# A linear-attention layer and two MLPs on one core: VectorE turns k as well as r and w

## The chip, the core and the metric

The kernel runs on one core of a Trainium2 chip. The core has TensorE (matrix products), VectorE, ScalarE and GpSimd (elementwise work), SyncE (here it only issues transfers), and 16 DMA engines that carry them. The engines run independently and wait for each other by semaphores; within an engine everything happens in the order written. The metric is the time of one execution in microseconds (us), less is better; the median of several runs counts.

## The reference

Three parts follow each other. The first is a recurrence over 768 steps for 4 batches of 8 heads of size 48, the second a dense MLP on 3072 tokens of 384 values, the third a mixture of 8 experts of which every token uses one.

```python
state = np.zeros((B, H, D, D))
for t in range(S):
    kt, vt, rt, wt = (k[:, :, t], v[:, :, t], r[:, :, t], w[:, :, t])
    cur = np.einsum('bhd,bhe->bhde', u[None] * kt, vt)
    y[:, :, t] = np.einsum('bhd,bhde->bhe', rt, state + cur)
    state = wt[:, :, :, None] * state + np.einsum('bhd,bhe->bhde', kt, vt)
# y as x, (tokens, 384)
h = x @ w_in                      # 384 -> 2048
x2 = np.maximum(0.01 * h, h) @ w_out
# experts: xn, en are x2 and expert_emb, normalized
logits = xn @ en.T / tau          # the router: 8 logits per token
expert_idx = np.argmax(logits, axis=1)
# out = softmax weight * relu(x2 @ w1[e]) @ w2[e], e = expert_idx
```

## The kernel before

**The attention.** The recurrence is worked off in 24 chunks of 128 steps (six for each batch, all heads together), numbered m = 0 to 23 in the code; this text counts the first to the 24th. For a chunk r, k and w are loaded with time along the partitions and must be turned, so that head values lie along the partitions and time along the columns. From the turned w VectorE makes running products (`decay_to`: `Fi`) and suffix products (`decay_from`: `Xi`) by scans; `decay_rk` multiplies the turned r and k by them into `Rh` and `Kt`. TensorE multiplies `Kt` by `Rh` (`scores`), VectorE masks the result (`mask`), and TensorE sums it with v and with the carried state (`sums`). GpSimd multiplies r, k and u for the diagonal (`products(m)` in its block), VectorE sums these into `bonus`, and ScalarE writes the diagonal (`diagonal`, eight operations on `As`).

**Who turns.** TensorE turns a chunk of 128 x 512 by four products with the identity into a PSUM bank. VectorE's `transpose` turns only blocks of 32 x 32 in place, so for it the blocks must be placed by the load: `load_blocks` does that with 16 small transfers. From the sixth chunk on w goes that way, from the tenth (`R_BLOCKED` = 9) r does too, half of its transfers issued by ScalarE's queue. k is turned by TensorE in all chunks (`turn_rk`), right behind a feature product.

**The MLP.** Tokens go in eight groups of three chunks (384 tokens). A group has 16 slots, f = 0 to 15. In slot n TensorE runs `feature(n)` (nine products of 384 columns, L1085) and `out_part(n - 2)` (nine, L1106). Between them ScalarE copies the feature out (`feature_copy`: `gw`), VectorE applies the leak (`leak`), ScalarE rounds it (`feature_hi`: `gh`) and VectorE takes the rest (`feature_lo(n - 1)`: `gl`), which stands first in VectorE's slot n. In ScalarE's slot n `feature_hi(n - 1)` stands first, then `feature_copy(n)`, then `diagonal`.

**How the two are mixed.** The three chunks of the next group are worked off inside the slots of the current one, by a table written by hand. `SLOTS` gives for the first, second and third chunk the slots of w's turn, of r and k's turn, of the scores and of the sums: (-2, -1, 1, 3), (3, 4, 6, 8) and (8, 9, 11, 13); negative slots are those at the end of the group before. VectorE's `decay_rk` comes in the slot after the turn, 0, 5 and 10, right behind `gl`. `BLOCK_SLOTS` gives VectorE's turn of w, `decay_to` and `decay_from`. The 24 router products of a group (`products(first, G, ...)`, L1809: each multiplies 384 values by an expert's vector and sums them) stand at the end of VectorE's slots. Their number per slot comes from a rule: none in slots 3, 4, 9 and 14, three in slots without attention work just before, else two, and the rest in slot 15; that gives 2, 0, 0, 2, 3, 2, 2, 0, 2, 3, 2, 3, 0 for slots 2 to 14 and 3 for slot 15.

**SyncE.** It issues nearly all transfers, in the order of the slots: the block loads of w (`next_w`, 16 transfers), r (`next_r`, eight), the plain r and k (`next_load`), v, and at a group's end the copies that fill the holes between heads of 48 in rows of 64 (`fill`). The chunk's plain k has three buffers, `m % NSLOT`.

## Time and profile before

| | us |
|---|---|
| median of 3 runs | 825.2 |
| lowest and highest | 823.98, 826.25 |
| the profiled execution | 825.9 |
| its span | 824.1 |
| TensorE busy | 807.5 |
| VectorE busy | 566.3 |
| ScalarE busy | 439.0 |
| GpSimd busy | 203.9 |

The times of single instructions come from the profiled execution; its span is what the trace covers. The attention lies in the first 475 us, almost all of it inside the MLP's slots, the experts follow from about 543 us on. A busy TensorE is not one at its peak, since matmuls overlap; what counts is the distance of their starts. The granted TensorE clock is full all along. In a timeline row stand start, duration, engine, line, operation, the tiles written and read, shapes and count; in brackets the engine's idle time before it and what ended it.

### The profile page before, as it was taken

To read this page: it belongs to the slowest core of one execution; us is meant where nothing else is said; L and a number is where in the kernel's file an instruction comes from. 1 tells how busy PE (TensorE), PEld (TensorE's weight loads), DVE (VectorE), ACT (ScalarE), POOL (GpSimd) and SP (SyncE) were. 2 spreads that over 40 slices of the span, in tenths; PEclk is the share of its full clock that TensorE was granted. 3 is DMA by queue.
4 is the path that set the end of the run, shared out by engine and by line. 5 is a ranking of instruction groups with operands and counts; after the bars stand their busy time and mean duration, and the time that the engine had idled before them with its cause. 6 is when DMAs were issued, how large, how long until landed. Compare 5 with 4: busy or idle time off the path is not lost. (4 is left out here: it accounts for less than half of the span.)

```text
span 824.1 us, 18207 instructions
## 1 busy us (share of the span) xinstructions
PE 807.5 (98%) x5573; PEld 757.5 (92%) x5573; DVE 566.3 (69%) x1330; ACT 439.0 (53%) x924; POOL 203.9 (25%) x288
## 2 busy tenths in 40 slices
PE   6999999999999999999999999999999999999996
PEld 6899999999999999999999999999989888998886
DVE  6879787789889878979979855735541512455463
ACT  6676564464375375465465444663643533565473
POOL 5611111112003002103112002303542422434423
PEclk9999999999999999999999999999999999999999
DMA  9975431347344243243330012215432414386291
GB/s 205 207 155 132 75 76 27 58 87 92 64 75 55 45 88 49 44 91 51 50 72 14 1 41 87 100 39 183 147 98 78 155 48 124 103 287 205 85 309 56
DMA packets 199866, 81.51 MB, mean 99 GB/s; under 512 B 170046, under 2 KB 187813, under 8 KB 199650
## 3 DMA queue, kind: packets, MB, share of 16 engines
q1 hardware_dynamic: 173682, 66.79, 34.1%
q0 software_dynamic: 4544, 10.85, 4.1%
q10 hardware_dynamic: 21552, 2.81, 2.5%
q8 instruction: 42, 0.69, 0.4%
q14 instruction: 46, 0.38, 0.2%
HBM read 115.85 MB, written 11.63 MB: 155 GB/s over the span
## 5 line engine op out<-in xcount | busy, mean ns | idle before, releaser
L1085 PE MATMUL bank<-xhl,WRh 128*128 128x384 f32 x768 | 219.1, 339 | 0.4 <-issue 0.2
L1085 PEld LDWEIGHTS bank<-xhl,WRh 128*128 128x128 f32 x768 | 141.3, 188 | 1.1 <-issue 1.1
L1106 PE MATMUL bank<-WRh,gh 128*128 128x384 f32 x384 | 135.8, 354 | 0.0
L1085 PE MATMUL bank<-xhl,WRl 128*128 128x384 f32 x384 | 130.0, 339 | 0.0
L1106 PE MATMUL bank<-WRh,gl 128*128 128x384 f32 x384 | 129.8, 338 | 0.0
L1106 PE MATMUL bank<-WRl,gh 128*128 128x384 f32 x384 | 129.7, 338 | 0.0
L1466 ACT CAST gh<-gw 128x384 fp32r<-128x384 f32 x128 | 65.4, 511 | 105.6 <-DVE gw L1789 87.4
L1460 ACT COPY gw<-bank 128x384 f32<-128x384 f32 x128 | 61.5, 480 | 107.3 <-PE bank L1085 106.8
L1796 DVE TENSOR_TENSOR gl<-gw,gh 128x384 fp32r<-128x384 f32 x128 | 71.7, 560 | 58.7 <-ACT gh L1466 52.8
L1964 DVE TENSOR_TENSOR hl<-bank,hh 128x512 fp32r<-128x512 f32 x56 | 36.1, 686 | 84.3 <-ACT hh L1501 83.9
L1789 DVE SCALAR_TENSOR_TENSOR gw<-gw 128x384 f32<-128x384 f32 x128 | 73.3, 572 | 18.7 <-ACT gw L1460 18.7
L795 POOL TENSOR_TENSOR St<-Sx,FL 128x256 f32<-128x256 f32 x20 | 12.3, 615 | 280.3 <-DVE Sx L1770 218.2
L1809 DVE CUSTOM_DVE_ANT_0 junk<-x2s,embb 128x384 bf16<-128x384 f32 x144 | 74.4, 558 | 0.0
L1106 PEld LDWEIGHTS bank<-WRh,gh 128*128 128x128 f32 x384 | 72.2, 188 | 2.3 <-issue 0.7
L1942 DVE TENSOR_TENSOR WRl<-stage,WRh 128x1536 fp32r<-128x1536 f32 x36 | 62.0, 1755 | 16.1 <-ACT WRh L1474 15.2
L1106 PEld LDWEIGHTS bank<-WRl,gh 128*128 128x128 f32 x384 | 72.3, 188 | 0.0
L1085 PEld LDWEIGHTS bank<-xhl,WRl 128*128 128x128 f32 x384 | 72.2, 188 | 0.0
L1106 PEld LDWEIGHTS bank<-WRh,gl 128*128 128x128 f32 x384 | 72.1, 188 | 0.0
L1194 PE MATMUL bank<-WRh,hh 128*128 128x384 f32 x184 | 63.9, 347 | 1.3 <-DVEq L1953 1.3
L1509 ACT ACTIVATE os<-bank,gcol 128x384 f32<-128x384 f32 x28 | 16.3, 583 | 87.4 <-PE bank L1194 80.9
L1194 PE MATMUL bank<-WRl,hh 128*128 128x384 f32 x184 | 62.0, 337 | 0.0
L1194 PE MATMUL bank<-WRh,hl 128*128 128x384 f32 x184 | 61.9, 336 | 0.0
(202 smaller groups left out, 1633.8 us busy)
## 6 DMA issues: line engine op xcount, KB each, us to landing
stage<-in_moe_w_dram SPq DMA_DIRECT2D x96, 768.0 KB
Kn<-in_k_dram SPq DMA_DIRECT2D x24, 192.0 KB, 3.4
Vn<-in_v_dram SPq DMA_DIRECT2D x24, 192.0 KB
x_moe<-x2s SPq DMA_DIRECT2D x24, 192.0 KB, 3.8
Rn<-in_r_dram SPq DMA_DIRECT2D x21, 192.0 KB, 2.7
wraw<-in_moe_w_out_dram SPq DMA_DIRECT2D x4, 768.0 KB, 7.6
eraw<-in_moe_w_dram SPq DMA_DIRECT2D x4, 768.0 KB, 9.0
Wn<-in_w_dram SPq DMA_DIRECT2D x152, 16.0 KB
```

Of the source, the lines that this page charges most:

```text
L795: pool.tensor_tensor(St[:], Sx[:], FL[:, m % GT, :].unsqueeze(2).to_broadcast([P, HP, HEAD_PAD]), ALU.mult).then_inc(s_st, 1)
L1085: mm = pe.matmul(bank[F_BANK[n % 2]][:, 0:GN], win(t_)[:, f // 4, k_, cols], xhl[G % 2][:, a, k_, :], start=(k_ == 0 and n_ == 0), stop=(k ...
L1106: mm = pe.matmul(bank[O_BANK[i]][:, 0:DM], a[:, z, cols], wout(t_)[:, f, :], start=(f == 0 and n_ == 0), stop=(f == FT - 1 and n_ == 2))
L1194: mm = pe.matmul(bank[R_BANK[s_]][:, 0:DM], h_[:, f, :], w_[:, f, :], start=(f == 0 and n_ == 0), stop=(f == FT2 - 1 and n_ == 2))
L1460: act.copy(gw[:, n % 2, :], bank[F_BANK[n % 2]][:, 0:GN]).then_inc(s_g0, 1)
L1466: act.copy(gh[:, n % GS, :], gw[:, n % 2, :]).then_inc(s_ghi, 1)
L1509: act.activation(os[:, s_, :], bank[R_BANK[s_]][:, 0:DM], ACT.Copy, scale=gcol[:, s_, :]).then_inc(s_o2e, 1)
L1789: dve.scalar_tensor_tensor(gw[:, z, :], gw[:, z, :], 0.01, gw[:, z, :], ALU.mult, ALU.max).then_inc(s_g1, 1)
L1796: dve.tensor_tensor(gl[:, n % GS, :], gw[:, n % 2, :], gh[:, n % GS, :].bitcast(F32), ALU.subtract).then_inc(s_glo, 1)
L1809: dve.tensor_tensor_reduce(junk[:, m % 2, :], x2s[:, i, :], embb[:, e, :], 1.0, 0.0, ALU.mult, ALU.add, logits[:, GT * G + i, e:e + 1]).th ...
L1942: dve.tensor_tensor(sel(w1l, w2l), src, sel(w1h, w2h).bitcast(F32), ALU.subtract).then_inc(s_elo, 1)
L1964: dve.tensor_tensor(lo, bank[H_BANK[a]][:], hi.bitcast(F32), ALU.subtract).then_inc(s_hlo, 1)
```

## The change

From the thirteenth chunk on (`K_BLOCKED` = 12) TensorE no longer turns k. VectorE's `decay_rk` turns it by `turn_k` behind r. Its blocks come in two steps: in slots 18 to 33 of the whole run (groups two and three), 32 transfers copy k's second half, two batches, from DRAM to DRAM into `k_packed`; then each chunk's blocks are loaded by four transfers (`next_kb`) into the second and third of k's buffers, which GpSimd clears once. The plain k, still needed by GpSimd's product, from then on has only the first buffer and is loaded by `next_k` when the product before is done. VectorE's turn of w for the second chunk of a group moves from slot 0 to slot -1, and ScalarE's check of w's range with it. The router products get a table of their own, `SHARE`. The last two apply to earlier chunks as well.

```diff
+    k_packed = nc.dram_tensor("k_packed", [B * NCH // 2, 4, HP * 4, 32, 32], F32, kind="Internal").ap()
...
+        K_BLOCKED = B * NCH // 2
+        def k_slot(m):
+            return m % NSLOT if m < K_BLOCKED else 0
+        def k_blocks(m):
+            return 1 + m % 2
...
-        BLOCK_SLOTS = ((-5, -3, -2), (0, 2, 4), (6, 8, 9))
+        BLOCK_SLOTS = ((-5, -3, -2), (-1, 2, 4), (6, 8, 9))
+        SHARE = {2: 1, 3: 0, 4: 0, 5: 1, 6: 5, 7: 3, 8: 2, 9: 0, 10: 1, 11: 5, 12: 3, 13: 3, 14: 0}
...
                 load_one(sp, m, 1)
+                if m < K_BLOCKED:
+                    load_one(sp, m, 2)
+            def next_k(m):
+                sp.wait_ge(s_rk, m)
+                if m == K_BLOCKED:
+                    sp.wait_ge(s_kT, m - 2)
                 load_one(sp, m, 2)
+            def pack_k(h, a):
+                o, top = divmod(32 * a, HEAD_PAD)
+                n_ = min(32, D - top)
+                for b in range(B // 2):
+                    sp.dma_start(k_packed[b * NCH:(b + 1) * NCH, a, 4 * h:4 * h + 4, :, 0:n_].rearrange("c b j i -> (b j) c i"),
+                                 k[B // 2 + b, 2 * h + o, :, top:top + n_].rearrange("(c t) i -> t c i", t=P)
+                                 ).then_inc(s_packed, 16)
+            def next_kb(m):
+                sp.wait_ge(s_packed, 16 * 4 * HP * (B // 2))
...
+                for a in range(4):
+                    n_ = min(32, D - 32 * a % HEAD_PAD)
+                    to = Kn[32 * a:32 * a + 32, k_blocks(m)].rearrange("p h d -> p (h d)").rearrange("p (x i) -> p x i", i=32)
+                    sp.dma_start(to[:, :, 0:n_], k_packed[m - K_BLOCKED, a, :, :, 0:n_].rearrange("x j i -> j x i")
+                                 ).then_inc(s_kblk[m % 2], 16)
...
+                for m in at(turn_w_at, n):
+                    if K_BLOCKED <= m + 1 < NC:
+                        next_k(m + 1)
+                if FT + 2 <= n < FT + 2 + 4 * HP:
+                    pack_k(*divmod(n - FT - 2, 4))
...
                         for m in at(turn_at, n):
-                            turn_rk(m)
+                            if m < K_BLOCKED:
+                                turn_rk(m)
...
+            def turn_k(m):
+                dve.wait_ge(s_kblk[m % 2], 16 * 4 * ((m - K_BLOCKED) // 2 + 1))
+                dve.wait_ge(s_mk, m)
+                dve.transpose(bank[k_bank(m)][:], Kn[:, k_blocks(m)].rearrange("p h d -> p (h d)")).then_inc(s_kT, 1)
...
                 if m >= R_BLOCKED:
                     turn_r(m)
+                if m >= K_BLOCKED:
+                    turn_k(m)
...
-                        light = not any(at(t_, n - 1) for t_ in (turn_at, score_at, sum_at))
-                        some = 0 if f in (4, 9, 14) or (f == 3 and G > 1) else 3 if light and f != 8 else 2
+                        some = SHARE.get(f, 0)
```

TensorE's order behind the feature product of slot 15, at the turn of the 22nd chunk's k, before:

```order
L1085 MATMUL bank<-xhl,WRl 128x384
L1085 MATMUL bank<-xhl,WRh 128x384
L972 MATMUL bank<-ident,Kn 128x128 x4
L1106 MATMUL bank<-WRh,gh 128x384
L1106 MATMUL bank<-WRl,gh 128x384
```

and now (`feature` is L1146 there, `out_part` L1167):

```order
L1146 MATMUL bank<-xhl,WRl 128x384
L1146 MATMUL bank<-xhl,WRh 128x384
L1167 MATMUL bank<-WRh,gh 128x384
L1167 MATMUL bank<-WRl,gh 128x384
L1167 MATMUL bank<-WRh,gl 128x384
```

The four products with the identity are gone; nothing takes their place.

VectorE's order from the last `gl` of a group on, at the 19th chunk, before:

```order
L1796 TENSOR_TENSOR gl<-gw,gh 128x384
L1685 STREAM_TRANSPOSE bank<-Rn 128x512
L1736 TENSOR_TENSOR Rh<-bank,Fi 128x512
L1742 TENSOR_TENSOR Kt<-bank,Xi 128x512
L1789 SCALAR_TENSOR_TENSOR gw<-gw 128x384
L1679 STREAM_TRANSPOSE Wn<-Wn 128x512
```

and now, from the `gl` one slot earlier (`gl` is L1866, `leak` L1859, w's turn L1741, the turns of r and k L1747 and L1754):

```order
L1866 TENSOR_TENSOR gl<-gw,gh 128x384
L1859 SCALAR_TENSOR_TENSOR gw<-gw 128x384
L1741 STREAM_TRANSPOSE Wn<-Wn 128x512
L1866 TENSOR_TENSOR gl<-gw,gh 128x384
L1747 STREAM_TRANSPOSE bank<-Rn 128x512
L1754 STREAM_TRANSPOSE bank<-Kn 128x512
L1806 TENSOR_TENSOR Rh<-bank,Fi 128x512
L1812 TENSOR_TENSOR Kt<-bank,Xi 128x512
```

k's turn stands between r's and `Rh`; w's turn for the next chunk has moved ahead of `gl`, where three router products stood before.

VectorE's order in slot 6, between the 20th and the 21st chunk, from the `leak` to the next `gl`, before:

```order
L1789 SCALAR_TENSOR_TENSOR gw<-gw 128x384
L1679 STREAM_TRANSPOSE Wn<-Wn 128x512
L1809 ISA junk,logits<-x2s,embb 128x384
L1809 ISA logits 128x1
L1809 ISA junk,logits<-x2s,embb 128x384
L1809 ISA logits 128x1
L1809 ISA junk,logits<-x2s,embb 128x384
L1809 ISA logits 128x1
L1796 TENSOR_TENSOR gl<-gw,gh 128x384
```

and now, without the `leak` (the router products are L1879, each with a row that reads its sum):

```order
L1741 STREAM_TRANSPOSE Wn<-Wn 128x512
L1879 ISA junk,logits<-x2s,embb 128x384
L1879 ISA logits 128x1
L1879 ISA junk,logits<-x2s,embb 128x384
L1879 ISA logits 128x1
L1879 ISA junk,logits<-x2s,embb 128x384
L1879 ISA logits 128x1
L1879 ISA junk,logits<-x2s,embb 128x384
L1879 ISA logits 128x1
L1879 ISA junk,logits<-x2s,embb 128x384
L1879 ISA logits 128x1
L1866 TENSOR_TENSOR gl<-gw,gh 128x384
```

There are five router products instead of three; slot 5 lost one and slot 7 got one.

## Rows read from the trace of the kernel before

**Rows 1.** the page's first part: busy time (share) xinstructions of each engine
```profile
PE 807.5 (98%) x5573; PEld 757.5 (92%) x5573; DVE 566.3 (69%) x1330; ACT 439.0 (53%) x924; POOL 203.9 (25%) x288
```

**Rows 2.** timeline, TensorE, turn of the 22nd chunk's k (start, us, engine line, tiles)
```profile
418.46 0.34 PE L1085 MATMUL bank<-xhl,WRh 128*128 128x384 f32 x1
418.64 0.60 PE L972 MATMUL bank<-ident,Kn 128*128 128x128 f32 x4
418.99 0.42 PE L1106 MATMUL bank<-WRh,gh 128*128 128x384 f32 x1
419.25 0.34 PE L1106 MATMUL bank<-WRl,gh 128*128 128x384 f32 x1
```

**Rows 3.** timeline, VectorE and TensorE, the third chunk: TensorE waits for Kt
```profile
23.72 0.68 DVE L1742 TENSOR_TENSOR Kt<-bank,Xi 128x512 f32<-128x512 f32 x1
...
24.54 0.38 PE L1011 MATMUL bank<-Rh,Kt 64*128 64x128 f32 x2 [0.97 <-DVE Kt L1742]
```

**Rows 4.** timeline, ScalarE, VectorE and TensorE, the 22nd chunk (first of its three)
```profile
419.68 2.45 ACT L1349 ACTIVATE As<-ident,bonus 128x128 f32<-128x128 f32 x8
...
422.04 0.50 ACT L1466 CAST gh<-gw 128x384 fp32r<-128x384 f32 x1
...
422.57 0.56 DVE L1796 TENSOR_TENSOR gl<-gw,gh 128x384 fp32r<-128x384 f32 x1 [0.57 <-ACT gh L1466]
423.04 0.72 DVE L1685 STREAM_TRANSPOSE bank<-Rn 128x512 f32<-128x512 f32 x1
423.80 0.69 DVE L1736 TENSOR_TENSOR Rh<-bank,Fi 128x512 f32<-128x512 f32 x1
424.40 0.68 DVE L1742 TENSOR_TENSOR Kt<-bank,Xi 128x512 f32<-128x512 f32 x1
...
425.51 0.38 PE L1011 MATMUL bank<-Rh,Kt 64*128 64x128 f32 x2
```

**Rows 5.** timeline, the 19th chunk (first of its three)
```profile
360.21 0.68 DVE L1742 TENSOR_TENSOR Kt<-bank,Xi 128x512 f32<-128x512 f32 x1
...
360.99 0.38 PE L1011 MATMUL bank<-Rh,Kt 64*128 64x128 f32 x2
```

**Rows 6.** timeline, the 23rd chunk (second of its three)
```profile
443.16 0.50 ACT L1466 CAST gh<-gw 128x384 fp32r<-128x384 f32 x1
...
445.53 0.68 DVE L1742 TENSOR_TENSOR Kt<-bank,Xi 128x512 f32<-128x512 f32 x1
...
446.59 0.38 PE L1011 MATMUL bank<-Rh,Kt 64*128 64x128 f32 x2
```

**Rows 7.** windows, us of each engine busy, between the 20th and the 21st chunk
```profile
380.00:397.00 17.00, 17.00 (x143) 16.10 (x142) 17.00 (x44) 7.86 (x20) 4.75 (x5) 1.00 0.41 64
```

**Rows 8.** timeline, two router products, and the 21st chunk (third of its three)
```profile
385.05 0.55 DVE L1809 CUSTOM_DVE_ANT_0 junk<-x2s,embb 128x384 bf16<-128x384 f32 x1
...
385.52 0.55 DVE L1809 CUSTOM_DVE_ANT_0 junk<-x2s,embb 128x384 bf16<-128x384 f32 x1
...
400.30 0.68 DVE L1742 TENSOR_TENSOR Kt<-bank,Xi 128x512 f32<-128x512 f32 x1
...
401.69 0.38 PE L1011 MATMUL bank<-Rh,Kt 64*128 64x128 f32 x2
```

**Rows 9.** timeline, the 24th chunk (third of its three)
```profile
465.66 0.68 DVE L1742 TENSOR_TENSOR Kt<-bank,Xi 128x512 f32<-128x512 f32 x1
...
467.23 0.38 PE L1011 MATMUL bank<-Rh,Kt 64*128 64x128 f32 x2
```

**Rows 10.** timeline, GpSimd product beside VectorE suffix scans, and such scans alone
```profile
394.29 1.01 POOL L784 TENSOR_TENSOR rku<-Rn,Kn 128x384 f32<-128x384 f32 x1
...
394.36 3.07 DVE L1723 TENSOR_TENSOR_SCAN Xi<-Wn,Xi,floor 128x127 f32<-128x127 f32 x4
...
414.92 1.60 DVE L1723 TENSOR_TENSOR_SCAN Xi<-Wn,Xi,floor 128x127 f32<-128x127 f32 x4
```

**Rows 11.** DMA queues in 395 to 401 us: packets, MB, share of 16 engines
```profile
q1 hardware_dynamic: 1511, 0.13, 18.1%
```

More of the change, by code:

```diff
@@ L196, in build @@
         s_pad = sem("s_pad")
+        s_kblk = [sem(f"s_kblk{i}") for i in range(2)]
+        s_padk = sem("s_padk")
+        s_packed = sem("s_packed")
         s_wT = sem("s_wT")
@@ L470, in load_one @@
         def load_one(eng, m, n_):
-            s_, (b, c) = (w_slot(m), r_slot(m), m % NSLOT)[n_], divmod(m, NCH)
+            s_, (b, c) = (w_slot(m), r_slot(m), k_slot(m))[n_], divmod(m, NCH)
             dst, src = nat[n_]
@@ L530, in next_load @@
                 load_one(sp, m, 1)
-                load_one(sp, m, 2)
+                if m < K_BLOCKED:
[4 more added lines that the diff above has]
+                    sp.wait_ge(s_kT, m - 2)
+                load_one(sp, m, 2)
+            def pack_k(h, a):
[7 more added lines that the diff above has]
+                sp.wait_ge(s_packed, 16 * 4 * HP * (B // 2))
+                if m < K_BLOCKED + 2:
+                    sp.wait_ge(s_padk, 1)
+                else:
+                    sp.wait_ge(s_kT, m - 1)
+                for a in range(4):
[3 more added lines that the diff above has]
+                                 ).then_inc(s_kblk[m % 2], 16)
             def next_w(m):
@@ L646, in mlp @@
                                 next_r(m + 2)
+                                next_kb(m + 2)
                         for m in at(turn_w_at, n - 4):
@@ L649, in mlp @@
                                 next_load(m + NSLOT)
+                        for m in at(turn_w_at, n):
+                            if m + 1 < NC:
+                                next_k(m + 1)
                     elif f == 0 and 0 < G < NG:
@@ L684, in _ @@
                         next_r(m + 2)
+                    if K_BLOCKED < m + 2 < NC:
+                        if m + 2 == K_BLOCKED + 1:
+                            next_kb(K_BLOCKED)
+                        next_kb(m + 2)
                 for m in at(turn_w_at, n - 4):
@@ L687, in _ @@
                         next_load(m + NSLOT)
+                for m in at(turn_w_at, n):
+                    if K_BLOCKED <= m + 1 < NC:
+                        next_k(m + 1)
+                if FT + 2 <= n < FT + 2 + 4 * HP:
+                    pack_k(*divmod(n - FT - 2, 4))
                 if n == 2 * FT + 4:
@@ L783, in products @@
                     pool.wait_ge(s_bo, m)
-                pool.tensor_tensor(rku[:], Rn[:, r_slot(m), :, 0:D], Kn[:, s_, :, 0:D], ALU.mult).then_inc(s_rk, 1)
+                pool.tensor_tensor(rku[:], Rn[:, r_slot(m), :, 0:D], Kn[:, k_slot(m), :, 0:D], ALU.mult).then_inc(s_rk, 1)
                 pool.wait_ge(s_rk, m + 1)
@@ L904, in mlp @@
                                 state(m)
+                        if n == turn_at[K_BLOCKED - 1] + 1:
+                            pool.wait_ge(s_kT, K_BLOCKED)
+                            pool.memset(Kn[:, 1:3].rearrange("p s h d -> p (s h d)"), 0.0).then_inc(s_padk, 1)
                         if n == turn_at[R_BLOCKED - 1] + 1:
```

## The prediction

> **What bounds the kernel now.** I read the page's first part, then the waits of TensorE, then the timeline around every place where the attention work enters the MLP's stream. TensorE is busy 98% of the span, VectorE 69%, ScalarE 53%, GpSimd 25% [rows 1]. TensorE's order is fixed, so a stretch of it gets shorter only by what is taken out of it. After its first slots TensorE names no wait until the last expert tiles. That does not say that the others are far behind: at each chunk TensorE multiplies the scores as soon as it comes to them, and how early VectorE had finished `Kt` by then is the distance that a change can use up. I call it the reserve: start of the score products (L1011) less the end of the `Kt` product (L1742).
>
> The reserve is what this case turns on. Chunks come in threes, one group of the MLP each; their scores stand in slots 1, 6 and 11. For the thirteenth to the 24th chunk the reserves are, in us: first of three 0.20, 0.56, 0.10, 0.43; second 0.21, 0.38, 0.21, 0.38; third 0.71, 0.81, 0.71, 0.89. Twelve in all, sum 5.59; five are shown: 425.51 - 424.40 - 0.68 = 0.43 [rows 4], 0.10 [rows 5], 0.38 [rows 6], 0.71 [rows 8] and 0.89 [rows 9]. When TensorE really waits for `Kt`, as at the third chunk, it starts 0.14 us after its end (24.54 - 23.72 - 0.68) [rows 3]. So a reserve of 0.14 is none, and the 19th chunk has none already.
>
> **The change part by part.** *The turn leaves TensorE.* It takes 418.99 - 418.64 = 0.35 us, and the matmul after it comes 0.26 instead of 0.18 after its predecessor, so 0.43 to 0.44 us [rows 2]. Twelve chunks: 12 x 0.44 = 5.3 us. This is all that the change can give, and only where nothing else is late.
>
> *The turn comes to VectorE,* between the turn of r and `Rh`, in the chain that ends in `Kt`. r's turn takes 0.72 us and `Rh` starts 0.76 after it; the next operation of 512 columns starts 0.60 after that [rows 4]. A second turn queued behind the first adds at least 0.60 + 0.60 - 0.76 = 0.44, if each hides the other's end, and at most another 0.76. I take 0.55, nearer to the low end, since the second turn needs no semaphore of the first and `Rh` no longer finds its own one fresh.
>
> Can VectorE begin this chain earlier? No. It starts with `gl` of the slot before, which waits for ScalarE's `gh`. At the 22nd chunk `gh` starts at 422.04, right behind the eight diagonal operations, 2.45 us from 419.68; VectorE waits 0.57 us for it after its three router products [rows 4]. Taking these products and adding w's turn there changes nothing. At the 23rd `gh` starts at 443.16 and all behind it, up to `Kt` at 446.21, is the chain itself [rows 6]. Both `gh` follow features that TensorE ran before the removed turn, so the 0.44 does not bring them forward either.
>
> *The sum at a chunk.* The scores now start 0.14 after `Kt`. Against before they start later by 0.55 + 0.14 - reserve. The 0.44 saved is not in it: TensorE arrives earlier by it and waits it away. If the result were negative by more than 0.44, TensorE would keep its whole saving; the largest reserve gives 0.69 - 0.89 = -0.20, so all twelve are decided by `Kt`. Over twelve chunks: 12 x 0.69 - 5.59 = +2.7 us.
>
> *Router products in other slots.* Between the second and the third chunk of a group before has 2, 3, 2 and 2 products (slots 5 to 8), the new table 1, 5, 3 and 2: two more. Products follow each other by 0.47 us [rows 8]: +0.94. Between these chunks VectorE has no hole: 17.00 of 17.00 us busy [rows 7], and its `leak` of slot 9 is what starts the third chunk's `gh`. So here the whole addition moves `Kt`. In the last group VectorE has more than 1 us in hand there, since ScalarE's diagonal ends later than the leak (its reserve of 0.89 [rows 9] is set by ScalarE). That leaves three groups: 3 x 0.94 = +2.8 us. The ends are 0 (the holes absorb it) and 4 x 0.94 = 3.8. The products taken from slots 2 and 10 to 15 come from stretches with waits for ScalarE and give nothing. The two groups before the thirteenth chunk get the new table too; their reserves at the third chunk are 0.82 and more, so I count 0 to 0.3 there, and take 0.
>
> *w's turn one slot earlier, and its check.* The turn, about as long as r's, leaves slot 0, behind which VectorE waits for ScalarE anyway, and fills half of the room that three products leave in slot 15 (3 x 0.47 = 1.4 us). ScalarE's check goes from slot 1 to slot 0, where ScalarE idles before `leak`. Cost 0, and up to 0.1 us a group if it should overlap.
>
> *Packing and loads.* 32 copies from DRAM to DRAM with 24,576 pieces of 64 and 128 B stand in SyncE's queue in slots 18 to 33. In a stretch with mostly such pieces, into the on-chip memory, 1511 packets took 18.1% of 16 engines over 6 us [rows 11]: 11.5 ns each, so 24,576 x 11.5 ns / 16 = 18 us of all engines, over 16 slots, one group: 425.51 - 360.99 = 64.5 us from one first chunk's scores to the next [rows 4, 5]. What stands behind them in the queue are loads that are made two chunks ahead. I take 0. The nearest end is 18 us if TensorE had to stand still for all of it, which the distance of the loads excludes; I keep 0 to 5 for a late hole copy at a group's start. The Trainium skill ("DMA: Bandwidth & Descriptors", section Specifications) says that below 512 B an engine reads, modifies and writes. No row here shows small pieces written to DRAM. By that rule the packing would cost about twice my 18 us of engine time, 36 of 64.5 us, and the sum would stay as it is.
>
> For each chunk k is loaded twice afterwards, once more in four transfers of 2048 pieces together: 2048 x 11.5 / 16 = 1.5 us of the engines in a third of a group, 21 us. The plain k has one buffer instead of three; it is asked for after GpSimd's last product and w's 16 issues, and has several us before the bonus sum. Price 0.
>
> *Sum:* 2.7 + 2.8 = +5.5 us. On the profiled execution's 825.9 us (span 824.1 and 1.8 around it) that is 831.4. The median of the runs is 0.7 lower, 825.2, so I forecast 830.7. Its own range comes from the two ends: 12 x (0.44 - 0.55) = -1.3, 12 x (0.76 - 0.55) = +2.5, -2.8 or +1.0 for the products: 826.6 to 834.2.
>
> **The rivals.** *The reserve suffices and TensorE keeps its saving.* For: no TensorE wait at all is named in these groups, VectorE is 69% busy [rows 1], and 15 turns of r are already made this way. Against: the reserves. All twelve turns would have to be hidden: 825.2 - 5.3 = 819.9.
>
> *Half the price.* Two mechanisms give it. Either the two products find room, leaving +2.7, or a collision goes away. In three of the four groups the suffix scans of the third chunk take 3.07 us beside GpSimd's product, against 1.60 alone [rows 10], 1.47 us more on the very chain that ends in `Kt`. The new single buffer of k could push GpSimd's product past these scans: 5.5 - 3 x 1.47 = +1.1. Against it: that product is released by a state that VectorE itself sums just before the scans, and k should have landed by then. So 826.3 to 827.9, most of it no measurable difference. The Trainium skill ("GPSIMD Engine Reference", section Specifications) has GpSimd share its SBUF interfaces with VectorE, with contention when VectorE's instruction has two SBUF inputs. The trace agrees with it at these scans: 3.07 against 1.60 us.
>
> *Slower by the transfers.* The hole copies of a group are issued in its slot 14 and TensorE needs them at the next slot 0, two slots of 64.5 / 16 = 4.0 us later. If packing keeps SyncE or the engines from them by over 6 us, TensorE stands at its feature product; once or twice 3 us on top of the +5.5 gives 836 or more. For: 24,576 of the smallest pieces and a DRAM write that no row shows. Against: SyncE waits for other engines most of that time, and the engines have room for 18 us in 64.5.
>
> **How the numbers follow.** Forecast 0.55, half price 0.20, saving kept 0.12, transfers 0.13. The measurement tells 0.3% (2.5 us) from no change. Faster by more: 0.12, the first rival alone. Within: three quarters of the half price and a little of the forecast's low end, 0.18. Slower: the rest, 0.70. Range 823.5 to 835.0: it leaves out the first rival and the upper half of the last.
>
> **What would show it.** Right: in the new profile TensorE waits at the scores of the thirteenth to the 24th chunk, released by `Kt`, 0.14 us after its end, with waits of about 0.44 + 0.69 - reserve: 0.7 to 1.0 us for first and second chunks, and 1.2 to 1.5 us for the third ones but 0.2 in the last group. `Kt` ends 0.55 later after `gl` than before. The 17 us stretch between second and third chunk grows by 0.9 on VectorE. Wrong: TensorE's scores start without idle time (first rival); the third chunks wait no longer than the others, or the scans no longer take 3 us (second); TensorE stands at a group's first feature with a DMA as releaser, in the second and third groups (third). My forecast fails too if ScalarE's `gh` comes earlier at slots 0 and 5, since I take it as fixed.

## The result, and the profile after

The changed kernel takes 842.5 us (median of 6 runs, 840.98 to 843.49) against 825.0 us before (6 runs), ratio 1.0211, interval 1.0201 to 1.0222. It is 17.5 us slower. The forecast had the sign right and the size wrong by three times: +5.5 us, 830.7, range to 835. One execution of experiment 2 (1124.9 us) and one of the kernel before beside experiment 13 (883.9) ran at a lower granted clock and are left out of all numbers. The profiled execution took 841.0 us, its span is 839.1 us, 15.0 above the span before; it is the fastest of the six, so the traces show less of the loss than the medians do.

The page's first part of the changed kernel, which answers to [rows 1]:

```profile
PE 807.0 (96%) x5525; PEld 757.1 (90%) x5525; DVE 581.2 (69%) x1342; ACT 437.3 (52%) x924; POOL 208.2 (25%) x289
```

TensorE has 48 matmuls less, the twelve turns of k, and is busy no shorter, although it has less to do: 10.2 us of its span now go by at half clock, and 8.2 of them are work. Its idle time comes on top. The waits of TensorE in the changed kernel (engine, what it would write, line, who released it: us in total, times, longest):

```profile
PE bank L1072 <- DVE Rh L1806: 8.6, 6, 1.8
PE bank L1146 <- DMA xhl<-xhl: 5.4, 1, 5.4
PE bank L1033 <- POOL tri L832: 5.1, 1, 5.1
PE bank L1072 <- issue: 2.5, 5, 0.5
PE bank L1072 <- DVE Kt L1812: 1.4, 2, 1.0
```

L1072 is the scores. Their waits are new, but for the last row, whose two lie in the early chunks; ten of the eleven stand at the thirteenth to the 24th chunk, one (0.98 us) at the 11th. (Releasers are inferred: VectorE ends `Kt`, L1812, about 0.1 us before each start.) L1146 is a feature product that stands 5.4 us for the hole copies, which fill the holes in the rows of its input `xhl`. The third row was there before and is the same.

The chain of the 22nd chunk in the timeline of the changed kernel, as in [rows 4] (start us, us, engine, line):

```profile
438.64 0.56 DVE L1866 TENSOR_TENSOR gl<-gw,gh 128x384 fp32r<-128x384 f32 x1 [1.49 <-ACT gh L1528]
439.12 0.72 DVE L1747 STREAM_TRANSPOSE bank<-Rn 128x512 f32<-128x512 f32 x1
439.75 0.68 DVE L1754 STREAM_TRANSPOSE bank<-Kn 128x512 f32<-128x512 f32 x1
440.34 0.67 DVE L1806 TENSOR_TENSOR Rh<-bank,Fi 128x512 f32<-128x512 f32 x1
440.93 0.67 DVE L1812 TENSOR_TENSOR Kt<-bank,Xi 128x512 f32<-128x512 f32 x1
...
441.70 0.83 PE L1072 MATMUL bank<-Rh,Kt 64*128 64x128 f32 x10 [0.49 <-issue]
```

From `gl` to the end of `Kt` it is 441.60 - 438.64 = 2.96 us, before 425.08 - 422.57 = 2.51: the second turn costs 0.45, the low end of my 0.44 to 0.76. Two turns in a row start 0.63 apart, and `Rh` follows the second after 0.59. The scores start 0.10 after `Kt`, not 0.14.

The third chunks are worse. The 21st chunk in the timeline of the changed kernel, beginning with the router products after the second chunk's scores:

```profile
393.72 1.16 PE L1072 MATMUL bank<-Rh,Kt 64*128 64x128 f32 x16 [1.38 <-DVE Rh L1806]
...
396.23 0.52 DVE L1879 CUSTOM_DVE_ANT_0 junk<-x2s,embb 128x384 bf16<-128x384 f32 x1
396.35 1.27 POOL L842 TENSOR_TENSOR rku<-Rn,Kn 128x384 f32<-128x384 f32 x1 [4.14 <-DMA Kn<-in_k_dram]
...
396.67 1.36 DVE L1879 CUSTOM_DVE_ANT_0 junk<-x2s,embb 128x384 bf16<-128x384 f32 x1
397.69 1.21 POOL L845 TENSOR_TENSOR rku<-rku,ub 128x384 f32<-128x384 f32 x1
...
397.96 1.35 DVE L1879 CUSTOM_DVE_ANT_0 junk<-x2s,embb 128x384 bf16<-128x384 f32 x1
...
409.03 3.06 DVE L1791 TENSOR_TENSOR_SCAN Xi<-Wn,Xi,floor 128x127 f32<-128x127 f32 x4
...
416.19 1.16 PE L1072 MATMUL bank<-Rh,Kt 64*128 64x128 f32 x16 [1.84 <-DVE Rh L1806]
```

From scores to scores it is 22.47 us; before it was 401.69 - 381.05 = 20.64. From `Kt` to `Kt` it is 22.47 against 20.14; VectorE has the same one hole in both, 0.58 us for the last `gh`. The difference: 0.45 for the turn, 0.94 for two products, about 0.8 for a collision, 0.1 left. GpSimd's product waits 4.14 us for the plain k, which has one buffer now, and then runs beside two router products. They take 1.36 and 1.35 us where the free one takes 0.52. The suffix scans of this chunk take 3.06 as before [rows 10], beside the next chunk's product: that collision has not gone, and where before had one long router product here there are two. The 15th chunk has two as well, the 18th one of 0.74 us.

The hole copies are late. SyncE's queue before (SPq: issue; start us, us for all, how many), from the broadcast (L691) to the copies (L466):

```profile
182.32 0.54 SPq L691 DMA_DIRECT2D x_moe<-x_moe  x1
186.22 8.64 SPq L487 DMA_DIRECT2D Rn<-in_r_dram  x8
...
221.03 1.91 SPq L466 DMA_DIRECT2D xhl<-xhl  x3
```

The same in the changed kernel:

```profile
187.16 6.67 SPq L749 DMA_DIRECT2D x_moe<-x_moe  x1
193.88 12.12 SPq L502 DMA_DIRECT2D Rn<-in_r_dram  x8
...
222.69 4.63 SPq L575 DMA_DIRECT2D Kn<-k_packed  x8
227.42 0.43 SPq L489 DMA_DIRECT2D Rn<-in_r_dram  x1
227.96 1.93 SPq L481 DMA_DIRECT2D xhl<-xhl  x3
```

They go out 6.9 us later, and TensorE meets them at the fourth group's first feature (timeline):

```profile
231.96 0.66 PE L1146 MATMUL bank<-xhl,WRh 128*128 128x384 f32 x1 [5.38 <-DMA xhl<-xhl]
232.42 0.52 PE L1146 MATMUL bank<-xhl,WRl 128*128 128x384 f32 x1
```

The windows of the changed kernel around its end (stretch, its length, busy time of PE, PEld, DVE, ACT and POOL, granted clock, DMA share, GB/s):

```profile
229.90:231.96 2.06, 0.00 (x1) 0.03 (x1) 2.06 (x4) 0.00 (x0) 0.00 (x0) 0.50 0.63 121
232.00:234.00 2.00, 2.00 (x6) 2.00 (x7) 0.71 (x2) 0.00 (x0) 0.00 (x0) 0.50 0.38 55
234.00:238.00 4.00, 4.00 (x17) 4.00 (x17) 0.56 (x1) 2.73 (x6) 0.00 (x0) 0.66 0.21 25
238.00:241.00 3.00, 3.00 (x30) 2.63 (x29) 1.69 (x6) 1.62 (x4) 0.00 (x0) 1.00 0.51 86
```

The clock falls to the lower level, 1.2 GHz, at 229.90, while TensorE still stands, and stays there for 6.83 us. In the first 2.06 nothing is lost by it; in the other 4.77 TensorE does half the work: 2.4 us more. The same happens behind the 1.84 us wait at 416.19, for 3.41 us, all of them work (1.7 more). Before had no such stretch between its start and its end.

The sum for the profiled execution: 5.4 (hole copies) + 11.7 (eleven waits at scores and two at masks, of 0.27 to 1.84 us) - 1.2 (TensorE's other waits, which are shorter than before) + 4.1 (clock) - 5.3 (turns gone) = 14.7, against 15.0 measured. The medians lie 17.5 apart; the other 2.5 us are in no trace.

### The profile page after: what moved, and what is told of

It is laid out like the page before. It is cut to its first block, busy times and chain, and to the rows that moved or that the text cites. A ratio compares the mean times of both kernels' runs of the same rounds, so it can differ in the third digit from the quotient of the medians.

```text
span 839.1 us, 18217 instructions
## 1 busy us (share of the span) xinstructions
PE 807.0 (96%) x5525; PEld 757.1 (90%) x5525; DVE 581.2 (69%) x1342; ACT 437.3 (52%) x924; POOL 208.2 (25%) x289
## 4 chain that ended last, share of the span: by engine, by line
PE 73%; DVE 9%; issue 5%; SPq 4%; ACT 4%; DMA 1%; ACTq 1%; DVEq 0%; POOL 0%; POOLq 0%
PE bank L1167 17%; PE bank L1146 17%; PE bank L1219 13%; PE bank L1255 13%; SPq L502 3%; PE bank L1236 3%; PE bank L1072 2%; PE bank L1100 2%; PE bank L1095 2%; DVE gw L1859 1%; DVE junk L1879 1%; PE bank L1201 1%; ACT As L1411 1%; DVE Xi L1791 1%; PE bank L1080 1%
## 5 line engine op out<-in xcount | busy, mean ns | idle before, releaser
L1146 PE MATMUL bank<-xhl,WRh 128*128 128x384 f32 x768 | 220.4, 341 | 5.6 <-DMA xhl<-xhl 5.4
L1146 PEld LDWEIGHTS bank<-xhl,WRh 128*128 128x128 f32 x768 | 142.2, 189 | 6.4 <-issue 6.4
L1167 PE MATMUL bank<-WRh,gh 128*128 128x384 f32 x384 | 135.9, 354 | 0.0
L1167 PE MATMUL bank<-WRl,gh 128*128 128x384 f32 x384 | 130.8, 341 | 0.0
L1167 PE MATMUL bank<-WRh,gl 128*128 128x384 f32 x384 | 130.7, 340 | 0.0
L1146 PE MATMUL bank<-xhl,WRl 128*128 128x384 f32 x384 | 130.5, 340 | 0.0
L1866 DVE TENSOR_TENSOR gl<-gw,gh 128x384 fp32r<-128x384 f32 x128 | 72.9, 570 | 58.8 <-ACT gh L1528 54.0
L1859 DVE SCALAR_TENSOR_TENSOR gw<-gw 128x384 f32<-128x384 f32 x128 | 73.1, 571 | 20.9 <-ACT gw L1522 20.9
L1879 DVE CUSTOM_DVE_ANT_0 junk<-x2s,embb 128x384 bf16<-128x384 f32 x144 | 77.5, 584 | 0.0
L1167 PEld LDWEIGHTS bank<-WRh,gh 128*128 128x128 f32 x384 | 73.0, 190 | 2.3 <-issue 0.5
L1167 PEld LDWEIGHTS bank<-WRl,gh 128*128 128x128 f32 x384 | 73.0, 190 | 0.0
L1167 PEld LDWEIGHTS bank<-WRh,gl 128*128 128x128 f32 x384 | 72.9, 190 | 0.0
L1146 PEld LDWEIGHTS bank<-xhl,WRl 128*128 128x128 f32 x384 | 72.8, 190 | 0.0
```

The costliest lines, as they stand in the source:

```text
L1146: mm = pe.matmul(bank[F_BANK[n % 2]][:, 0:GN], win(t_)[:, f // 4, k_, cols], xhl[G % 2][:, a, k_, :], start=(k_ == 0 and n_ == 0), stop=(k ...
L1167: mm = pe.matmul(bank[O_BANK[i]][:, 0:DM], a[:, z, cols], wout(t_)[:, f, :], start=(f == 0 and n_ == 0), stop=(f == FT - 1 and n_ == 2))
L1859: dve.scalar_tensor_tensor(gw[:, z, :], gw[:, z, :], 0.01, gw[:, z, :], ALU.mult, ALU.max).then_inc(s_g1, 1)
L1866: dve.tensor_tensor(gl[:, n % GS, :], gw[:, n % 2, :], gh[:, n % GS, :].bitcast(F32), ALU.subtract).then_inc(s_glo, 1)
L1879: dve.tensor_tensor_reduce(junk[:, m % 2, :], x2s[:, i, :], embb[:, e, :], 1.0, 0.0, ALU.mult, ALU.add, logits[:, GT * G + i, e:e + 1]).th ...
```

## The experiments

In each the text names the kernel that the edit starts from; "less" without a name means against the changed kernel. "Late broadcast" is the 1152 KB copy `x_moe<-x_moe` (L749) put off to where SyncE has few chunk loads left. Lines of later kernels differ from these by a few.

**1. The broadcast two groups later, all else as changed.**
```diff
-                if n == 2 * FT + 4:
+                if n == 4 * FT + 4:
```


> The changed kernel with one edit: the zero-fill of the last token rows (one DRAM-to-DRAM transfer of 1152 KB), which stands in SyncE's queue at slot 4 of the third group, moves to slot 4 of the fifth. Theory A (the hole copies come late because SyncE's queue is full: the broadcast's 6.7 us and the block loads of r slowed behind it, 12.1 us, stand ahead of them, and the 5.4 us stall then drops TensorE's clock): the wait of 5.4 us at 232 us goes, the stretch at half clock behind it goes, and the time falls by 7 to 9 us, to about 834 us. Rival B (the packing's and the block loads' own issues fill the queue): the wait shrinks by less than 2 us and the time stays above 840. Rival C (the clock's loss is no result of that stall): the wait goes but the clock row still shows the half level near 230 us, gain 5.4 or less.

834.6 us (ratio 1.0114, 1.0097 to 1.0131): 7.9 less. The wait at 232 us is gone, but 2.07 us for `xhl` appear at 360.3, with half clock behind them: the broadcast had only moved to another group's copies. The waits at the scores stay.

**2. The table of before.** The number of router products by slot and w's turn as before, k's turn and the early broadcast as changed.
```diff
-        BLOCK_SLOTS = ((-5, -3, -2), (-1, 2, 4), (6, 8, 9))
+        BLOCK_SLOTS = ((-5, -3, -2), (0, 2, 4), (6, 8, 9))
...
-                        some = SHARE.get(f, 0)
+                        light = not any(at(t_, n - 1) for t_ in (turn_at, score_at, sum_at))
+                        some = 0 if f in (4, 9, 14) or (f == 3 and G > 1) else 3 if light and f != 8 else 2
```


> The changed kernel with the router products' old rule and w's turn of the second chunk back in slot 0; k's turn stays on VectorE. Theory A (the two more products between the second and the third chunk are worth 0.94 us of wait in three groups): waits before the scores of the third chunks shrink from 1.6 to 1.8 us to about 0.8, those of first and second chunks stay, and the time falls by 2 to 4 us against the changed kernel, to about 839. Rival (the new table relieves the first and second chunks by as much as it costs the third): their waits grow and the time is the same within 1 us.

833.9 us (median of three; ratio 1.0095, 1.0068 to 1.0122): 8.6 less, where I expected 2 to 4. The third chunks wait 0.47, 0.46 and 0.86 instead of 1.84, 1.63 and 1.84. The stall at 232 us is gone too, although the broadcast is early: its issue takes 0.53 us here, and `xhl` is waited for 0.16 us at one place. So the stall takes both, the early broadcast and the new table with w's turn. A wait of 1.96 us at 211.7, at the twelfth chunk, is new, with 3.41 us at half clock behind it; ScalarE, whose queue issues half of r's transfers, needs 3.10 us for two of them there, 0.81 in experiment 13.

**3. Before, with the packing alone** (the copies into `k_packed`, which nothing reads).
```diff
+            def pack_k(h, a):
...
+                if FT + 2 <= n < FT + 2 + 4 * HP:
+                    pack_k(*divmod(n - FT - 2, 4))
```


> The kernel before plus the packing alone: the 32 transfers from DRAM to DRAM in slots 18 to 33, which nothing reads. Theory A (the packing alone leaves SyncE enough room; it is the packing together with the next block loads and the broadcast that makes the hole copies late): TensorE waits 0 to 1 us more, 825 to 826 us. Rival B (packing alone is what delays them): a TensorE wait for the hole copies of 2 us or more and a time of 828 or more.

826.4 us (ratio 1.002, 1.0008 to 1.0033), 1.5 over before; one new wait of 1.21 us at 210, at the twelfth chunk, and one of 0.41 at the 19th. The first starts in ScalarE's queue: two of r's transfers take 2.80 us to issue instead of 0.81, `gh` is late behind them, and VectorE waits 2.52 us for it instead of 0.54. The copies cost 1.5 us, not the 18 us that I had estimated as their engine time.

**4. Turn of 32 of 512 columns,** with the rest of k's turn left out:
```diff
-                dve.transpose(bank[k_bank(m)][:], Kn[:, k_blocks(m)].rearrange("p h d -> p (h d)")).then_inc(s_kT, 1)
+                dve.transpose(bank[k_bank(m)][:, 0:32], Kn[:, k_blocks(m)].rearrange("p h d -> p (h d)")[:, 0:32]).then_inc(s_kT, 1)
```


> The changed kernel, but VectorE's turn of k covers 32 of the 512 columns, so the rest of k's turned values is left out: the operation, its waits and loads stay, its length goes. Theory A (the length of the turn sits on the chain that ends in Kt): each of twelve waits before the scores shrinks by about 0.5 us, the time falls by 5 to 6 us against the changed kernel, to about 837. Rival (the waits come from elsewhere, late k blocks or ScalarE): less than 2 us.

837.3 us (ratio 1.0145, 1.0128 to 1.0162): 5.2 less. `gl` to the end of `Kt` is 2.52 again, as before. Waits at most first and second chunks vanish (0.80 and 0.74 us stay at the 19th and the 20th); the third ones still wait 1.40 us each, so what is behind them is not the turn. The wait for the holes is 6.45 us here, and 10.24 us are at half clock, as many as in the changed kernel. The 5.2 us are near 12 x 0.45, but the two profiled spans differ by 2.7 only, so this does not prove the price of a turn.

**5. Turns early, nearly the table of before, broadcast two groups later.** The slots between second and third chunk have 2, 3, 2 and 2 products, as before, and w's turn is back in slot 0. r's and k's turns go to the end of VectorE's slot before, ahead of `gl`, whose `gh` ScalarE is still making.
```diff
-        BLOCK_SLOTS = ((-5, -3, -2), (-1, 2, 4), (6, 8, 9))
+        BLOCK_SLOTS = ((-5, -3, -2), (0, 2, 4), (6, 8, 9))
+        SHARE = {2: 2, 5: 2, 6: 3, 7: 2, 8: 2, 10: 2, 11: 4, 12: 3, 13: 4}
...
-                if n == 2 * FT + 4:
+                if n == 4 * FT + 4:
...
-                if m >= R_BLOCKED:
-                    turn_r(m)
-                if m >= K_BLOCKED:
-                    turn_k(m)
...
+                    if not first:
+                        for m in at(turn_at, n):
+                            if m >= R_BLOCKED:
+                                turn_r(m)
+                            if m >= K_BLOCKED:
+                                turn_k(m)
```


> The changed kernel with the broadcast in the fifth group, w's turn of the second chunk back in slot 0, a product table 2: 2, 5: 2, 6: 3, 7: 2, 8: 2, 10: 2, 11: 4, 12: 3, 13: 4 (no product in slots 3, 4, 9, 14, 15), and VectorE's turns of r and k moved from behind gl to the end of the slot before, where VectorE waits for ScalarE's gh anyway. Theory A (the turns cost because they stand on the chain gl to Kt, which is 2.96 us with both): the chain shrinks to about 1.8 us, TensorE's waits before the scores all but vanish, the saving of 5.3 us comes out in part: 821 to 825 us. Rival (the end of the slot before is as full, and gl moves back by the turns' length): waits before the scores of 0.3 us or more stay in most chunks, time 827 or more.

824.1 us (ratio 0.998, 0.9965 to 0.9995). `gl` to the end of `Kt` is 1.72 to 1.76 (1.97 at the 15th chunk, whose `gl` runs beside GpSimd). Of the waits 1.91 us for `xhl` at 355 are left, with 3.4 us of half clock behind, and 0.38 at 402.

**6. Before, with the new table and w's turn one slot earlier,** k still on TensorE.
```diff
-        BLOCK_SLOTS = ((-5, -3, -2), (0, 2, 4), (6, 8, 9))
+        BLOCK_SLOTS = ((-5, -3, -2), (-1, 2, 4), (6, 8, 9))
+        SHARE = {2: 1, 3: 0, 4: 0, 5: 1, 6: 5, 7: 3, 8: 2, 9: 0, 10: 1, 11: 5, 12: 3, 13: 3, 14: 0}
...
+                        some = SHARE.get(f, 0)
```


> The kernel before with the new table of router products and w's turn one slot earlier, nothing else: k stays with TensorE. Theory A (the table's two more products reach Kt of the third chunks, whose reserve of 0.7 to 0.8 us takes most of them; w's loads come earlier in SyncE's queue): waits of 0.1 to 0.4 us before the scores of third chunks, 825 to 827 us. Rival B (the table alone carries a large part of the loss): 829 us or more. Rival C (the table helps when k is not turned by VectorE): below 824.

827.7 us (ratio 1.0028, 1.0018 to 1.0039), 2.5 over before. That it is near my 2.8 is luck, since it did not come about as I had it. At the third chunks `Kt` follows `Kt` after 21.06 us instead of 20.14, so the two products do cost 0.92 on VectorE; TensorE's reserve of 0.71 takes up all but 0.14. What costs are three second chunks, the 11th, the 17th and the 23rd, with waits of 0.99, 1.00 and 1.04 us, and 0.31 at the 19th. The timeline of this kernel before the 17th:

```profile
314.63 1.91 DVE L1797 TENSOR_TENSOR gl<-gw,gh 128x384 fp32r<-128x384 f32 x1 [1.69 <-ACT gh L1467]
315.09 1.02 POOL L785 TENSOR_TENSOR rku<-Rn,Kn 128x384 f32<-128x384 f32 x1
...
318.60 0.46 PE L1012 MATMUL bank<-Rh,Kt 64*128 64x128 f32 x3 [1.00 <-DVE Rh L1737]
```

`gl` takes 1.91 instead of 0.56 us beside GpSimd's product: the same collision, on the very operation that starts the chain. The 11th chunk, which I had counted as free, has this wait in the changed kernel too.

**7. Turns early, new table kept, broadcast two groups later:** experiment 5 without its `SHARE` and its slot for w's turn.
```diff
-                if n == 2 * FT + 4:
+                if n == 4 * FT + 4:
...
-                if m >= R_BLOCKED:
-                    turn_r(m)
-                if m >= K_BLOCKED:
-                    turn_k(m)
...
+                            if m >= R_BLOCKED:
+                                turn_r(m)
+                            if m >= K_BLOCKED:
+                                turn_k(m)
```


> The changed kernel with the broadcast in the fifth group and the turns of r and k moved to the end of the slot before; the product table and w's slot stay as the change has them. Against the run with the broadcast alone moved (834.6) theory A expects the waits of the first and second chunks to vanish and those of the third to shrink from 1.8 to about 1 us: 827 to 830 us. If the table costs nothing once the turns are off the chain, this comes within 1 us of the run with the other table. Rival: no better than 833.

829.2 us (ratio 1.0047, 1.003 to 1.0063), 5.1 over experiment 5. It has 5.23 us of waiting for `xhl` at 362, where experiment 5 has 1.91, and half clock twice; the first, at 65 us, lies behind a wait for weights that has nothing to do with the change. So the table and the queue of SyncE are not independent.

**8. Before, with sixteen copies from DRAM to DRAM put ahead of the third group's hole copies.** They are transfers into `k_packed`, which nothing reads.
```diff
+            def pack_k(h, a):
...
+                if n == 2 * FT + 13:
+                    for i_ in range(8):
+                        pack_k(*divmod(i_, 4))
```


> The kernel before with 16 extra transfers from DRAM to DRAM (a third of k copied once and part of it, read by nothing), put into SyncE's queue right ahead of the hole copies of the third group, so that these are issued some 7 us late as in the changed kernel. Nothing else is changed, no turn and no table. Theory A (late hole copies stall TensorE at the fourth group's first feature, and the granted clock falls behind such a stall): one TensorE wait of 3 to 6 us with the copies as releaser near 226 us, a half-clock stretch of 3.4 or 6.8 us behind it, and a time longer by the wait and half of that stretch: 830 to 834 us. Rival (the clock fell for another reason in the changed kernel, such as VectorE's turns or the waits before scores): the wait comes, but the clock row stays full, 829 or less.

831.5 us (ratio 1.0089, 1.007 to 1.0109), 6.4 over before. The copies go out at 224.76 instead of 221.03, TensorE stands for them once and has no other new wait:

```profile
228.42 0.66 PE L1099 MATMUL bank<-xhl,WRh 128*128 128x384 f32 x1 [2.48 <-DMA xhl<-xhl]
```

The windows of this kernel from there, with the granted clock in the third column from the end:

```profile
228.00:230.00 2.00, 1.58 (x5) 1.61 (x6) 1.97 (x4) 0.00 (x0) 0.00 (x0) 0.56 0.65 117
230.00:232.00 2.00, 2.00 (x9) 2.00 (x8) 0.30 (x1) 0.33 (x1) 0.00 (x0) 0.58 0.22 28
```

The clock is at the lower level for 3.41 us from 228.25 on. So a queue that is 3.7 us late costs 2.5 us of waiting and 1.6 us of clock, 4.1. The profiled execution's span is 3.1 us longer, the median 6.4; the sizes don't close, the mechanism shows.

**9. Experiment 5 with the broadcast behind the last chunk loads.**
```diff
-                if n == 4 * FT + 4:
+                if n == 6 * FT + 4:
```


> The early turns (r's and k's block turns at the head of VectorE's slot), with the broadcast of the fourth group's columns moved behind the last chunk loads that SyncE issues near the holes' copies. My theory (order on VectorE plus order on SyncE explain all of the loss): the 1.91 us wait for xhl at a group's first feature and the 3.4 us of half clock behind it go, TensorE waits in total under 1.5 us, and the time is 820 to 822 us, faster than before by 0.4 to 0.6%. Rival (the packed turn is itself worth nothing, or the extra DMA traffic costs elsewhere): 824 to 826 us.

821.3 us (ratio 0.9955, 0.9941 to 0.9969): faster than before by 4.0 us and than experiment 5 by 2.8. The first part of this kernel's page:

```profile
PE 802.7 (98%) x5525; PEld 753.2 (92%) x5525; DVE 576.4 (70%) x1342; ACT 438.1 (53%) x924; POOL 211.9 (26%) x289
```

The 21st chunk's chain in its timeline:

```profile
395.76 0.71 DVE L1747 STREAM_TRANSPOSE bank<-Rn 128x512 f32<-128x512 f32 x1
395.87 0.51 ACT L1528 CAST gh<-gw 128x384 fp32r<-128x384 f32 x1 [0.94 <-DVE gw L1855]
396.39 0.68 DVE L1754 STREAM_TRANSPOSE bank<-Kn 128x512 f32<-128x512 f32 x1
396.98 0.53 DVE L1862 TENSOR_TENSOR gl<-gw,gh 128x384 fp32r<-128x384 f32 x1
397.44 0.67 DVE L1802 TENSOR_TENSOR Rh<-bank,Fi 128x512 f32<-128x512 f32 x1
398.03 0.67 DVE L1808 TENSOR_TENSOR Kt<-bank,Xi 128x512 f32<-128x512 f32 x1
...
398.80 0.60 PE L1072 MATMUL bank<-Rh,Kt 64*128 64x128 f32 x6 [0.38 <-issue]
```

Both turns stand in the time in which `gl` would wait for `gh`; `gl` starts 0.56 later than it could (396.42, if it followed `gh` as elsewhere), and from `gl` to the end of `Kt` it is 1.72 us instead of 2.96: 1.24 are off the chain. TensorE is busy 4.8 us less than before, close to the 5.3.

**10. As changed, with the late broadcast.**
```diff
-                if n == 2 * FT + 4:
+                if n == 6 * FT + 4:
```


> The changed kernel with only the broadcast moved to the same late place. My theory: no wait for xhl at any group's first feature, while the waits at the scores stay as they were (0.5 us, and 1.6 to 1.8 in the third chunks); half clock is left only behind those. 831 to 834 us. Rival (the copies are late because of the packing's traffic, not because of the broadcast): a wait of 2 us or more for xhl stays somewhere, 836 to 841 us.

837.1 us (ratio 1.0152, 1.0136 to 1.0167). No wait for `xhl`; r's eight loads are issued in 8.77 us, and the hole copies at 221.74. The waits at the scores stay, 1.79 and 1.84 at two third chunks, and behind both there is half clock for 3.41 us:

```profile
341.28 1.16 PE L1072 MATMUL bank<-Rh,Kt 64*128 64x128 f32 x16 [1.79 <-DVE Rh L1806]
...
409.97 1.16 PE L1072 MATMUL bank<-Rh,Kt 64*128 64x128 f32 x16 [1.84 <-DVE Rh L1806]
```

The mechanism is as I expected, the time 3 us above my 831 to 834: the profiled execution has 835.3, three others 836.0 to 838.5, and what they lose more no trace shows. Nor does my theory explain that its median is 2.5 over experiment 1; the profiled executions of the two are only 0.3 apart.

**11. Late broadcast, and no plain k from the thirteenth chunk on.**
```diff
-                load_one(sp, m, 2)
...
-                pool.tensor_tensor(rku[:], Rn[:, r_slot(m), :, 0:D], Kn[:, k_slot(m), :, 0:D], ALU.mult).then_inc(s_rk, 1)
+                pool.tensor_tensor(rku[:], Rn[:, r_slot(m), :, 0:D], (Kn[:, k_slot(m)] if m < K_BLOCKED else Rn[:, r_slot(m)])[:, :, 0:D], ALU.mult).then_inc(s_rk, 1)
```


> The kernel with the late broadcast, and from the thirteenth chunk on without the load of plain k: GpSimd's product r x k takes r twice there, so k is left out of the bonus of those chunks. My theory (the single buffer of plain k delays GpSimd's product until it runs beside VectorE's router products, which then take 1.35 us and not 0.55): the products are back at 0.55 us, the waits at the third chunks' scores fall from 1.8 to about 1.0 us, and the time is 2 to 3 us below the kernel with the late broadcast alone. Rival (the two extra products are the whole of it): waits and time stay within 0.5 us.

831.0 us (ratio 1.0074, 1.0059 to 1.009), 6.1 below experiment 10, twice what I expected. No router product is long any more, and the third chunks wait 0.76, 0.39 and 0.75 instead of 0.71, 1.79 and 1.84, the 14th and the 20th 0.51 each instead of 1.18 and 1.12. In exchange GpSimd's product falls on `gl` at two second chunks, which wait 1.65 instead of 0.52 and 0.75:

```profile
315.28 1.70 DVE L1865 TENSOR_TENSOR gl<-gw,gh 128x384 fp32r<-128x384 f32 x1 [1.72 <-ACT gh L1527]
315.71 0.83 POOL L841 TENSOR_TENSOR rku<-Rn 128x384 f32<-128x384 f32 x1
```

The loads of the plain k are gone too, and what that does to the queue is not separated. The waits fall by 1.9 us in all, and both stretches of half clock are gone, 3.4 us: 5.3 of the 5.4 us by which the span is shorter.

**12. Before, with everything of experiment 9 but k's move:** late broadcast, early turn of r, the same table.
```diff
+        SHARE = {2: 2, 5: 2, 6: 3, 7: 2, 8: 2, 10: 2, 11: 4, 12: 3, 13: 4}
...
-                if n == 2 * FT + 4:
+                if n == 6 * FT + 4:
...
-                if m >= R_BLOCKED:
-                    turn_r(m)
...
+                    if not first:
+                        for m in at(turn_at, n):
+                            if m >= R_BLOCKED:
+                                turn_r(m)
```


> The kernel before, k turned by TensorE throughout, with everything else of the best version: late broadcast, early block turn of r, the same table of router products. It tells what k's move itself brings. My theory: k's move frees TensorE of 12 x 0.44 = 5.3 us, so this one is 3 to 5 us above the best version, 824 to 826 us. Rival (the gain of the best version comes from the order alone): equal to it within 0.5 us.

825.0 us (ratio 0.9994, 0.9985 to 1.0003). Against 821.3 k's move is worth 3.7 us, of 5.3 at most, and the order by itself nothing.

**13. k's turn in its place, table of before, late broadcast.** It gives the turn's price alone, which was still open. It is experiment 2 with this:
```diff
-                if n == 2 * FT + 4:
+                if n == 6 * FT + 4:
```


> The changed kernel's turn and packing with the kernel before's router products and w's turn, and the broadcast late. My theory (the turn lays 0.44 us on VectorE's chain and 0.10 us to the scores, twelve times, less reserves of 5.59 us that TensorE had, so 12 x 0.54 - 5.59 = 0.9 us; packing 1.4 us as measured apart; GpSimd's product, late by the single buffer of plain k, adds a collision in some chunks, up to 3 us): 827 to 830 us, and the third chunks' waits under 1 us. Rival (the turn's own price is the larger part and the table only a small one): 832 to 835 us, near the run with the table of before and the early broadcast, and then the table's price against the late broadcast alone (837.1) is under 4 us.

829.2 us (ratio 1.0055, 1.0041 to 1.0069), 4.5 over before. The waits at the scores are 0.35 to 1.45 us, with no half clock between start and end. In the profiled executions TensorE's waits are 9.6 us longer than before; less the 5.3 saved that makes 4.3 of the 5.1 us by which the span is longer. The collision with GpSimd's product, late by the single buffer, also meets the router's small operations, ahead of the 14th chunk:

```profile
234.53 1.05 DVE L1920 SCALAR_TENSOR_TENSOR r<-logits,rtau,q 128x24 f32<-128x24 f32 x1
234.53 1.02 POOL L842 TENSOR_TENSOR rku<-Rn,Kn 128x384 f32<-128x384 f32 x1 [29.25 <-DMA Kn<-in_k_dram]
...
236.05 0.67 DVE L1923 TENSOR_TENSOR r<-r,q 128x24 f32<-128x24 f32 x1
...
253.29 1.16 PE L1072 MATMUL bank<-Rh,Kt 64*128 64x128 f32 x16 [1.34 <-DVE Rh L1806]
```

Before these two took 0.24 and 0.18 us. Taken with experiment 10 the new table, with w's turn one slot earlier, costs 837.1 - 829.2 = 7.9 us. The two were never run apart.

## Why the prediction was wrong

The medians make a ladder of differences: +4.5 over before with k's turn and its packing (13); +7.9 with the new table and w's turn (10); +5.4 with the early broadcast (the changed kernel, 842.5). Of the 4.5 the packing is 1.5 (3). The steps don't simply add: with the table of before the early broadcast costs 833.9 - 829.2 = 4.7 (2 and 13), by another wait. The forecast had 2.7, 2.8 and 0.

**The sum at a chunk: right in its form, near in its number by luck.** 4.5 - 1.5 = 3.0 us for the turn with its loads, forecast 2.7. But the turn costs 0.45 and not 0.55, the signal 0.10 and not 0.14, which gives 12 x 0.55 - 5.59 = 1.0. The trace of experiment 13 shows where the other 2 come from. By these sizes, a chunk's wait is 0.44 + 0.45 + 0.10 less its reserve, 6.3 us for the twelve; measured are 8.9. The excess is at the 14th, 15th, 18th and 20th chunk, 0.56 to 0.74 us each, and ahead of each of them VectorE's operations are long beside GpSimd's product. In the changed kernel TensorE waited at ten of the twelve chunks (the first hides in the stall for the holes, the last has no wait), so there the saved 0.44 was waited away. The first and second chunks waited 0.5 to 1.4 us where I had 0.7 to 1.0; the third ones 1.6 to 1.8 for 1.2 to 1.5; the last none for 0.2.

**"Price 0" for the single buffer of plain k: failed,** by the 2 us above. I had it land several us before the bonus sum, and so it does. But what counts is when GpSimd's product runs, since VectorE's operations beside it take 1.35 for 0.55, 1.9 for 0.56, 1.05 for 0.24 and 3.06 for 1.60 us. My second rival used this collision and saw only that it might go away.

**"Router products in other slots", +2.8: failed.** The step said that the whole addition moves `Kt` at third chunks, 3 x 0.94, and stopped there. The 0.92 on VectorE was measured (6), and with k on VectorE it arrives: in the profiled executions of 10 and 13 the scores from the thirteenth to the 24th chunk take 245.4 and 240.5 us, and of the 4.8 us more 2.3 are in the third chunks' stretches. What the step left out is that the waits reach 1.8 us there, with half clock behind two of them: about 3 us are in the stretches with half clock. It also took the earlier groups as free, and `gl` at the 11th chunk runs beside GpSimd's product, 1.00 us of waiting (10). The long router products are no price of the table: 13, with the table of before, has five of them between second and third chunks, 10 has four. The other 3 us between the medians are not explained.

**Packing, "I take 0": failed, by the third rival.** Alone the copies cost 1.5 us (3). The larger part was SyncE's order: two blocked k loads of 4.63 us of issue, the broadcast and the loads behind it slowed from 9.2 to 18.8 us, all ahead of the hole copies. I gave it 0.13 and +3 to +5 us; moving one transfer gives back 5.4 (10) or 7.9 (1). I had it in the second and third groups; it came at the fourth group's first feature. And I had put the harmless lateness at 6 us: in experiment 8 copies that are 3.7 us late stall TensorE for 2.5, so it is about 1.2.

**The clock was in no term.** All my waits were priced at their own length.

**ScalarE's `gh` as fixed: right, and the way out.** Since `gh` doesn't come earlier, VectorE has 0.6 us before it. The turns fill this and push `gl` back by 0.56 us, which is still less than the 1.24 that they take off the chain (9).

## What to carry to other kernels

Work that moves to an engine with "room" costs nothing only where that engine waits for somebody: look for the idle time named in front of an operation on the chain, and put the new work there, not behind it. Before pricing a table of slots, list what a second engine does at the same time in the same memory, and what a buffer taken away does to its start. And go through every in-order queue from the new entries to the next transfer with a deadline; a stall there can cost more than its length, by a slower clock behind it.

## What the runs showed that I had not expected

- Around the end of a TensorE wait the granted clock was 0.5 for 3.41, 6.83 or 10.24 us (1.84, 5.38 and 6.45 us of waiting), the beginning of the long ones inside the wait. The length of the wait alone doesn't tell: 5.23 us in experiment 7 had 3.41, and the 1.84 us wait at 281.75 in the changed kernel had none.
- An operation of VectorE of 128x384 takes 1.35 instead of 0.55 us beside GpSimd's 128x384 product, with `gl` up to 1.95 for 0.56 (6), an operation of 128x24 up to 1.05 for 0.24, and GpSimd's own product 1.2 to 1.4 for 1.0.
- In the changed kernel the issue of one 1152 KB copy from DRAM to DRAM took 6.67 us instead of 0.54, and the eight loads behind it 12.12 instead of 8.64. With the packing alone (3) it was 0.53 and 11.75, with the table of before (2) 0.53 and 13.93, with the broadcast elsewhere (10) 8.77 for the loads. What makes the copy's own issue long is open.
